# Routing inside the attention block, and expert tiles gathered from token order

## The reference

```python
q_rot, k_rot = rotate(q), rotate(k)                  # rotary embedding
attn = softmax(q_rot @ k_rot.T / 8)                  # per batch and head, 576 x 576
x = (attn @ v)                                       # -> 2304 x 512
xn, en = x / |x|, expert_emb / |expert_emb|
logits = xn @ en.T / tau                             # 8 experts
idx = argmax(logits); gate = max(softmax(logits))
y[idx == e] = gate * (relu(x[idx == e] @ w1[e]) @ w2[e])   # 512 -> 1024 -> 512
h = y @ w_in                                         # 512 -> 2048
out = (h - tanh(h)) @ w_out                          # 2048 -> 512
```

## Time and profile before

| | before |
|---|---|
| time, median of 3 runs | 1116.12 us (1115.24 to 1118.18) |
| the profiled execution's own time | 1110.96 us |
| span of the profile | 1109.1 us |
| PE busy | 985.1 us, 89% of the span |
| DVE, ACT, POOL busy | 595.5, 582.4, 415.7 us |
| mean granted TensorE clock | 0.964 |

### The profile page before, as it was taken

How to read it: one execution, slowest core, us unless ns; L and a number is a source line. 1 busy time by engine, 2 the same in 40 slices (tenths; PEclk the granted TensorE clock), 3 DMA queues, 4 the chain that set the end, 5 groups by cost and what they waited for, 6 DMA issues and landing times. The chain is left out here.

```text
span 1109.1 us, 18954 instructions
## 1 busy us (share of the span) xinstructions
PE 985.1 (89%) x5604; PEld 871.1 (79%) x5605; DVE 595.5 (54%) x1195; ACT 582.4 (53%) x1273; POOL 415.7 (37%) x246
## 2 busy tenths in 40 slices
PE   1899999999995039999999976999999999999996
PEld 1899899989984038888888855888989889899895
DVE  4677777777773731111111104777666666666764
ACT  1677777777772632222322214666565565655653
POOL 3998788887510428309948305000000000000000
PEclk9999999999998569999999997999999999999999
DMA  8777777767503455314433106111000000000001
GB/s 236 192 207 197 219 189 202 206 186 205 145 21 90 169 188 202 97 47 151 152 123 113 38 30 200 58 48 48 1 19 10 0 28 0 13 15 0 28 2 28
DMA packets 63077, 113.82 MB, mean 103 GB/s; under 512 B 20032, under 2 KB 24640, under 8 KB 61120
## 3 DMA queue, kind: packets, MB, share of 16 engines
q1 hardware_dynamic: 52352, 92.62, 29.0%
q10 hardware_dynamic: 7808, 11.31, 3.2%
q0 software_dynamic: 2880, 9.44, 2.5%
HBM read 60.58 MB, written 24.41 MB: 77 GB/s over the span
## 5 line engine op out<-in xcount | busy, mean ns | idle before, releaser
L1429 PE MATMUL hd_ps<-y_hi,w_hi 128*128 128x384 f32 x384 | 130.9, 341 | 7.8 <-DVE g_sb L1599 7.8
L1429 PE MATMUL hd_ps<-y_lo,w_hi 128*128 128x384 f32 x384 | 129.6, 338 | 0.0
L1429 PE MATMUL hd_ps<-y_hi,w_lo 128*128 128x384 f32 x384 | 129.3, 337 | 0.0
L1499 ACT ACTIVATE mag<-hd_ps 128x384 f32<-128x384 f32 x96 | 47.3, 493 | 152.2 <-PE hd_ps L1429 149.8
L617 DVE TENSOR_REDUCE neg_max<-ps 128x1 f32<-128x576 f32 x144 | 108.1, 751 | 31.4 <-PE ps L373 28.9
L633 DVE TENSOR_TENSOR pt_lo<-ps,pt_hi 128x512 fp32r<-128x512 f32 x144 | 99.2, 690 | 43.3 <-ACT pt_hi L538 41.7
L538 ACT ACTIVATE pt_hi<-ps 128x512 fp32r<-128x512 f32 x144 | 86.8, 604 | 58.9 <-PE ps L420 57.5
L1447 PE MATMUL o_ps<-w_hi,g_hi 128*128 128x512 f32 x288 | 115.0, 399 | 2.2 <-DVE g_lo L1608 2.2
L1447 PE MATMUL o_ps<-w_hi,g_lo 128*128 128x512 f32 x288 | 114.3, 397 | 0.0
L1608 DVE TENSOR_TENSOR g_lo<-g_sb,g_hi 128x384 fp32r<-128x384 f32 x96 | 53.5, 558 | 112.3 <-ACT g_hi L1514 112.3
L1447 PE MATMUL o_ps<-w_lo,g_hi 128*128 128x512 f32 x288 | 113.5, 394 | 0.0
(11 more groups left out here) (208 smaller groups left out, 2429.8 us busy)
## 6 DMA issues: line engine op xcount, KB each, us to landing
w_stage<-in_w SPq DMA_DIRECT2D x32, 512.0 KB, 3.6
raw_qk<-in_qk SPq DMA_DIRECT2D x14, 1152.0 KB, 6.1
k_hh<-qk_hi SPq DMA_DIRECT2D x64, 144.0 KB, 2.8
k_ll<-qk_lo SPq DMA_DIRECT2D x64, 144.0 KB, 2.9
sorted_rows<-zeros SPq DMA_DIRECT2D x28, 256.0 KB, 6.2
x_row<-sorted_rows ACTq DMA_DIRECT2D x20, 256.0 KB, 2.7
y_rows<-y_row ACTq DMA_DIRECT2D x20, 256.0 KB, 2.1
q_st<-qk_hi SPq DMA_DIRECT2D x32, 144.0 KB, 3.0
```

The lines of the kernel that those rows point to most:

```text
L1429: op = nc.tensor.matmul(hd_ps[f % 2][:, 0:G], w[:, c, cols], y[:, c, :], start=c == 0 and h == 0, stop=c == DC - 1 and h == 2)
```

## The change

- **Routing goes into the attention block.** The function `routing` is gone. DVE runs `route()` after the last pair, PE its count, its ranks and 18 new matmuls, ACT the squares (the first three inside the last pair but one), SP the loads of the first expert's w1. One wait of all engines for each other is left between attention and experts, in place of two.
- **Router constants first.** The embedding norm is computed at the very start, and the fold matrix is scaled by it. Two loads are put at the head of ACT's queue, a Sqrt at the head of ACT's work, and a chain of DVE ahead of `rope_first`.
- **The chain is rebuilt**: scans in place of doubling additions, bit operations, expert-major layout. `first_set` releases the first w1 loads before positions are made.
- **Gather in place of scatter.** `x_rows` holds x in token order, stored by SP (`store_main`, `store_tail_rows`). DVE builds one-hot matrices, PE multiplies them by the token numbers (split in two parts) and so gets `gid`, the token of each slot. POOL gathers each tile's rows with it: tile 0 in the attention block, tiles 1 to 20 at the start of the experts block, ahead of the second expert's weight split, and tiles 21 to 24 behind it. `token_rows` has 21 tiles (`HELD`); the clears of `sorted_rows` and the loads of `x_row` are gone.
- **Tail rows** are loaded earlier; the last pair's go by four short DMAs.
- **First expert.** DVE makes the low part of w1 in the experts block while `up_first` runs (order: x_hi w_hi, x_lo w_hi, x_hi w_lo); SP loads each chunk of w2 when DVE has freed its place; ACT splits w2 inside tile 0, after the gate's Exp. The gate is computed in the experts block.
- **PE's tiles 1 to 15 are written out** in place of the hardware loop. The identity matrix is loaded once.
- In `dense` only buffers move.

```diff
+HELD = T + -(-T * H * E // D)          # 21
+AHEAD = HELD
 # attention, start
+            act.dma_start(emb_sb[:], a["emb_t"].rearrange("(c p) e -> p c e", p=P)).then_inc(emb_in, 16)
+            act.dma_start(tau_sb, a["tau"].partition_broadcast(P)).then_inc(emb_in, 16)
             act.dma_start(cos_sb[:, 1, :], a["cos"]).then_inc(tables_in, 16)
...
+            act.wait_ge(emb_clamped, 1)
+            nc.scalar.activation(emb_n[:, 1, :], emb_n[:, 0, :], ACT.Sqrt).then_inc(emb_root, 1)
...
+            dve.wait_ge(emb_in, 32)
+            nc.vector.tensor_tensor(emb_sq[:], emb_sb[:], emb_sb[:], ALU.mult).then_inc(emb_squared, 1)
+            chain(nc.vector.reciprocal(inv_tau, tau_sb))
+            dve.wait_ge(emb_summed, 1)
+            nc.vector.tensor_scalar(emb_n[:, 0, :], norm_ps, 1e-30, None, ALU.max).then_inc(emb_clamped, 1)
+            dve.wait_ge(emb_root, 1)
+            newton(chain, nc, emb_n[:, 2, :], emb_n[:, 1, :], emb_n[:, 0, :], emb_n[:, 3, :])
+            chain(nc.vector.tensor_scalar(emb_n[:, 4, :], emb_n[:, 2, :], inv_tau, None, ALU.mult))
             dve.wait_ge(tables_in, 32)
             rope_first(1, first_k_in, first_k_mult, first_k_done)
 # attention, SP's end
+            body(PAIRS - 4, 0, more_raw=False)
+            for b in range(B - 1):
+                store_main(b, slice(0, D))
...
             sp.wait_ge(x_done, PAIRS * 2)
+            pass_tail(PAIRS - 1, 1, "logits", last_logits)
+            store_main(B - 1, late)
+            pass_tail(PAIRS - 1, 1, "rows", last_in)
+            sp.wait_ge(last_in, 32)
+            store_tail_rows(B - 1, late)
+            sp.wait_ge(first_set, 1)
+            expert = sp.value_load(plan[0:1, FIRST, 0:1], min_val=0, max_val=E - 1)
+            for c in range(UP):
+                sp.dma_start(staged(stage, c), weight_chunk(a["w1"], a["w2"], expert, c)).then_inc(w_in0[c], 16)
 # attention, DVE's end (the core of route)
+                add_heads(slice((B - 1) * FULL, T))
...
+                nc.vector.tensor_tensor(chosen, base[:], best[:].unsqueeze(1).to_broadcast(wide),
+                                        ALU.is_equal).then_inc(hot_done, 1)
+                dve.wait_ge(counted, 1)
+                chain(nc.vector.tensor_tensor_scan(flat, total_ps[:, 1:1 + E * T], mask, 0.0, ALU.add, ALU.mult))
...
+                nc.vector.tensor_scalar(plan[:, SLOT, 0:E], sum_i, 1, None, ALU.bitwise_and).then_inc(first_set, 1)
...
+                chain(nc.vector.tensor_tensor(tile_eq[:], split_pos[:, 0, :].unsqueeze(2).to_broadcast(in_tile),
+                                              marks.unsqueeze(1).to_broadcast(in_tile), ALU.is_equal))
+                for i in range(2):
+                    nc.vector.tensor_tensor(tile_ids[:, :, i, :], tile_eq[:],
+                                            token[:, i, :].unsqueeze(2).to_broadcast(in_tile), ALU.mult)
+                for i in range(3):
...
+                    nc.vector.tensor_tensor(slot_hot[:, at, :], split_pos[:, 1, at].unsqueeze(2).to_broadcast(some),
+                                            iota.unsqueeze(1).to_broadcast(some), ALU.is_equal).then_inc(slots_hot, 1)
+                dve.wait_ge(ids_ready, 1)
...
+                nc.vector.tensor_tensor(gid[:], id_sum[:], id_ps[:, MT:2 * MT], ALU.add).then_inc(gid_done, 1)
 # attention, POOL's end
+            pool.wait_ge(gid_done, 1)
+            pool.wait_ge(sq_done, T)
+            pool.wait_ge(x_stored, 16 * 2 * (B + 1))
+            gather_x(nc, x_dram, rows, gid, 0).then_inc(first_x, 16)
 # experts
             for c in range(UP, CHUNKS):
+                sp.wait_ge(w_split, c - RING + 1)
                 sp.dma_start(staged(stage, c), weight_chunk(w1, w2, expert, c)).then_inc(w_landed[c % RING], 16)
...
+            for t in range(1, AHEAD):
+                gather(t)
+            pool.wait_ge(w_split, CHUNKS)
+            with pool.Fori(0, 1) as before:
+                next_set(before)
...
-            with pe.Fori(1, MT - 2) as t:
-                with pe.If(t < fourth + 2):
+            for t in range(1, T - 2):
+                tile(t)
+            for t in range(T - 2, MT - 2):
+                with pe.If(fourth > t - 2):
                     tile(t)
...
             take_x(1)
+            act.wait_ge(scaled, 1)
+            nc.scalar.activation(work[:], work[:], ACT.Exp).then_inc(exp_done, 1)
+            tile(0, start=True, split=True)
```

More of the change, by code:

```diff
@@ L598, in _ @@
+            act.wait_ge(last_in, 32)
+            square(T - 1)
+            act.wait_ge(first_set, 1)
+            slot = act.value_load(plan[0:1, SLOT, 0:1], min_val=0, max_val=1)
+            for c in range(UP):
+                act.wait_ge(w_in0[c], 16)
+                nc.scalar.activation(chunk_of(w_hi, slot, c), stage[:, c, :], ACT.Identity).then_inc(w_hi0, 1)
+            act.wait_ge(sq_done, T)
+            nc.scalar.activation(norm[:, 1, :], norm[:, 0, :], ACT.Sqrt, bias=least)
         @block.vector
@@ L1224, in take_y, with tile @@
                 act.dma_start(y_dram[bass.ds(t * P, P), :], y_row[:]).then_inc(y_stored, 16)
-            def tile(t, start=False, second=False, turn=True, load_next=True, last=False):
+            def tile(t, start=False, second=False, turn=True, last=False, split=False):
                 for f in range(2):
@@ L1233, in tile @@
                     take_y(t - 1, second)
+                if split:
+                    slot = act.value_load(plan[0:1, SLOT, 0:1], min_val=0, max_val=1)
+                    for c in range(UP, CHUNKS):
+                        act.wait_ge(w_landed[c % RING], 16)
+                        nc.scalar.activation(chunk_of(w_hi, slot, c), stage[:, c % RING, :],
+                                             ACT.Identity).then_inc(first_hi, 1)
                 if not last:
@@ new lines, in build @@
+        plan, _ = sb("plan", [P, ROWS, MT], I32)
+        first_x = ctx.enter_context(nc.semaphore("first_x"))
+        with ExitStack() as inner:
+            raw_l = inner.enter_context(nc.sbuf_tensor("raw_l", [P, E, T], F32))
+            norm = inner.enter_context(nc.sbuf_tensor("norm", [P, 4, T], F32))
+            stage = inner.enter_context(nc.sbuf_tensor("w_stage", [P, RING, CHUNK], F32))
+            attention(nc, a, first_x, w_at, nc.sbuf_base - 4 * RING * CHUNK, rows, tail_dram, x_dram, y_dram, id_sb, stage,
+                      w_hi, w_lo, pos_i, plan, gid, raw_l, norm)
+            experts(nc, a["w1"], a["w2"], a["w_in"], first_x, rows, x_dram, y_dram, id_sb, stage, w_hi, w_lo, gid, plan,
+                    raw_l, norm, gate)
@@ L1677 @@
+        dense(nc, a["w_out"], id_sb, y_dram, w_hi, w_lo, rows[:, 0:T, :], rows[:, T:HELD, :].rearrange("p t d -> p (t d)"),
+              pos_i, gate, out)
 def kernel(q, k, v, moe_expert_emb, moe_tau, moe_w1, moe_w2, moe2_w_in, moe2_w_out):
```

819 lines of the change are left out of this document (429 added, 390 removed).

## The result

The changed kernel took 1100.32 us in the median of 4 runs (1099.45 to 1104.31), the kernel before 1116.5 beside it (1115.24 to 1118.18): a ratio of 0.986 [0.983, 0.989]. The forecast was 1091 with a range of 1085 to 1099. The direction was right, and the time lies 1.3 us above the range: of 24.9 us forecast, 16.2 came.

A forecast was written before the change was run, and what follows sets the result against it. PE was taken to bound attention and expert tiles, with a shortenable hole between them. Start +5.5, squares +0.3 and earlier `down(0)` −30.7 sum to −24.9 us: 1116.12 becomes 1091.2 us, range 1085 to 1099.

The forecast's parts named there:

- The start: Kernel's start: norm chain and added loads delay DVE's first rotation and first scores, +5.5 us; ACT's squares in attention +0.3.
- Routing: Between attention and experts: the rebuilt chain opens experts at 369.8 in the old clock instead of 399.2, 29.4 us gained.
- Experts' start: From the experts' opening to tile 0's w2 product: `down(0)` at 390.2 in the old clock instead of 420.93, −30.7 us.
- rival 1: w2 handover: w2 late beside gathers costs 2.4 to 5 us, routing 2 to 4 more; about 1098 us, chance 0.15.
- half rate: w2 handover, a bound: w2 at half its rate beside 20 gathers lands last at 392.6, old clock, losing 5 us.
- Tiles of 12.5 us as before: Expert tiles, a sign of being right: PE takes 12.5 us a tile, unchanged.
- Rival 3: Expert tiles: PE's fifteen written-out tiles each begin with a gap awaiting instructions, 36 us in all, 1127 us; chance 0.03.
- Dense is unchanged: Dense block, after the expert tiles: its time stays the same, adding nothing to the sum.
- The base: Whole kernel: −24.9 us applied to the profiled 1110.96 gives 1086.1; the median, 5.16 above it, gives 1091.2.

The follow-up runs named there:

- e5: The changed kernel run again unaltered, second series, against the kernel before (1111.78 us): 1090.67 us, ratio 0.9811.
- e12: The changed kernel run again unaltered, third series, against the kernel before (1110.66 us): 1089.59 us, ratio 0.9811.
- e18: The changed kernel run again unaltered, fifth series, against the kernel before (1111.23 us): 1090.63 us, ratio 0.9816.
- e14: The changed kernel run again unaltered, fourth series (chip 10), against the kernel before (1116.56 us): 1101.23 us, ratio 0.9871.

## Why the prediction was wrong

Two things that the sum put at nothing were not nothing: the end of PE's written-out tiles, 6.4 us and more on every chip, and the stalls of PE and ACT in the experts' start and in dense, which came only where the kernel before takes 1116 us and with w2's late landing cost 9.4 us in the comparison. The terms one by one:

**The start: right in size, in part by luck.** +5.5 and +0.3 were forecast, +5.59 measured at attention's end. But the first rotation came at 13.89 and not at 12.5, and 2.1 us of its lateness were given back before the first scores, not 0.4. The reason given was only half of it: the tables, asked for behind `tau` and `emb_t`, landed at 13.2, so moving the chain alone would have won little.

**Routing: right** within 0.2 us from DVE's restart (355.71) to the opening of the experts (375.61). One pair of errors cancels: the last one-hot ended at 368.05 and not at 368.5, and then DVE waited 2.39 us for PE, not 1.6. The scan took 0.46 us beside 0.31 for a plain operation of 144 elements; by the Trainium skill's page on DVE's opcodes ("DVE: opcode table, instruction layouts, handler registers and perf-mode slots", section 6) a scan runs at half throughput, and the trace agrees. The drain of 1.38 us that the Trainium skill's page "ScalarE: Activation LUTs" (What ACT_TABLE_LOAD costs) adds to a switch of tables does not show: Exp starts at 389.17, 1.29 us behind the load's start.

**Experts' start: right on faster chips, 2.4 us off in the comparison.** w2 was to land by 385.4 + 5.8 = 391.2 and `down(0)` to start at 396.0. In e5, e12 and e18 the last packet of w2 ends at 390.95 to 391.62 and `down(0)` starts at 395.72, 395.97 and 397.22. In the comparison rival 1 came true in its mechanism, w2 late beside the gathers: 395.02, half of the way to the 398.4 of its half rate, and 2.4 us lost. But e12 and e14 have the same gathers and w2 in time, so the gathers alone don't make it late. Inside `down(0)` 2.8 us more went in gaps of PE that the prediction didn't have, and in e14 `down(0)` was 3.7 us late though w2 had landed at 391.25. The prediction had priced the gathers for POOL's issue and for w2's rate, and put what they do to the issue of PE and ACT at nothing; the cause of that stays open.

**"Tiles of 12.5 us as before": wrong at their end.** This is the step that failed on every chip. Rival 3 named the mechanism, PE starving for instructions, and looked for it at the head of each tile, where it isn't (12.35 us a tile). It is at the one place where PE leaves its straight code, whose cost the sum had at nothing: 6.4 us more in the last three tiles than before on a faster chip (39.15 in e12 against 32.70), 7.8 in the comparison; with the conditions in each other they take 31.98. The argument against the rival, attention's written-out bodies, had no skipped code in it. The Trainium skill's page "Runtime: NRT & Kernel Launch" (Instruction fetch mechanics) says that instructions come in blocks of 16 KiB one after another and that a taken branch out of the blocks at hand waits for a fetch; the packets here are 16 KB, and one jump, two and five leave 0.65, 4.65 and 5.6 to 6.6 us. What it adds, that full unrolling is preferred, has its price here where written-out pieces are skipped.

**"Dense is unchanged": right on faster chips** (436.9 us from `y_gated` to the end in e12, 437.4 before), 4.2 us short in the comparison.

**The base, and luck.** On a faster chip the sum is −24.9 + 6.4 − 2.8 for the shorter tiles = −21.3, and 20.6 to 21.1 were measured. In the comparison's profile 2.4 us at the handover, 2.8 in `down(0)`, 4.2 in dense and 1.4 more at the tiles' end make it −10.5, and the spans say −10.2. The 16.2 of the medians come about because the kernel before was itself slower there: 1116.5 beside the 1110.96 of its profile. The prediction took that 5.16 us as an addition that the changed kernel would carry too. The changed kernel's profile took 1100.70 where 1086.1 was forecast, 14.6 us off, and its median 1100.32 where 1091.2 was, 9.1 off: the addition hid 5 us of the miss. Where the kernel before loses these 5 us no trace shows, since none was taken of it at that level.

## What to carry to other kernels

Code that a run may skip can cost TensorE where it is skipped. Here five jumps, each past one written-out piece, idled it for 5.6 to 6.6 us, and one jump past all of them for 0.65; so put conditions on consecutive written-out pieces into each other, and look for instruction packets around the place. A move of small DVE operations to a place where DVE is free must look at POOL as well. And a step that only sends requests, here 20 gathers from POOL's queue, isn't always free beside engines that the plan wants full: on chip 10 the stalls of PE and ACT moved when the gathers were moved. So time a change on more than one chip before its last per cent is believed, and look at which level the kernel before had when its profile was taken.

## What was not expected of the hardware

- On chips where the kernel before takes 1116 us, a dense run of gathers goes with one matmul of PE in 2 to 3 us and with ACT standing for up to 17.37 us; where it takes 1111 us, PE is busy for 15.00 of 15 us in the same stage. SP is slowed too: its register moves at w2's handover took up to 0.71 us in the comparison's profile and 0.03 in e12. Instructions, semaphores, the recording or something else: not settled.
- TensorE lost more than the gap itself: a granted clock of 0.63 on average in the 8 us from 612 in e5, and 2.2 us more than the gap in the last three tiles.
- DVE operations of 8 elements a partition took 2.20 and 2.58 us beside POOL's sums. Those with one input did not (0.20). The Trainium skill's page "SBUF — State Buffer" (SBUF: two separate sides) has DVE operations with two SBUF inputs and GpSimd operations that read SBUF lock each other out; the trace agrees.
